# First three query tiles of an attention block: the value tiles become the stationary operand

## The reference

```
scores = q @ k.T / sqrt(64); keep = (key < n_sink) | (0 <= pos_q - pos_k < window)
a = exp(scores - max); a = a / (sum(a) + 1e-9); x = a @ v        # per head
h = max(x @ w_in, 0);  x = (h * h) @ w_out
h = x @ w2_in;  g = P(h) / Q(h);  out = g @ w2_out               # P, Q: polynomials in h and |h|
```

## Time and profile before

| | |
|---|---|
| median of 3 runs | 636.86 us (636.72 to 638.67) |
| profiled execution | 636.6 us, its span 634.9 us |
| PE busy | 625.2 us, 98% |
| DVE, ACT, POOL busy | 449.7, 380.2, 353.8 us (71%, 60%, 56%) |
| chain that ended last | PE 83%, DVE 12%, ACT 2%, POOL 1% |
| DMA over the span | 67 GB/s |

### The profile page before, as it was taken

One profiled execution on the slowest core, in us unless ns is written; L12 is line 12 of the kernel. 1 busy time (PEld: TensorE's weight loads), 2 busy tenths in 40 slices (PEclk: granted clock), 3 DMA queues, 4 the chain that ended last, 5 costly groups with the idle time before them and its releaser, 6 DMA issues.

```text
span 634.9 us, 10375 instructions
## 1 busy us (share of the span) xinstructions
PE 625.2 (98%) x3716; PEld 586.4 (92%) x3716; DVE 449.7 (71%) x705; ACT 380.2 (60%) x859; POOL 353.8 (56%) x431
## 2 busy tenths in 40 slices
PE   8999999999999999999999999999999999999997
PEld 6889999999999999999999998888999999999995
DVE  5655655354655656443567799998999989998995
ACT  4755666365444545443222576688777877778774
POOL 6899865122333334330222478777777677777773
PEclk9999999999999999999999999999999999999999
DMA  8776311052021401000444210021001110001001
GB/s 257 234 242 233 115 42 42 1 167 83 1 84 43 141 23 62 18 2 3 130 133 131 79 57 2 1 101 51 1 1 43 70 39 0 1 2 51 1 0 56
DMA packets 28972, 43.50 MB, mean 69 GB/s; under 512 B 4080, under 2 KB 19440, under 8 KB 28400
## 3 DMA queue, kind: packets, MB, share of 16 engines
q1 hardware_dynamic: 28912, 42.74, 20.7%
HBM read 36.44 MB, written 6.29 MB: 67 GB/s over the span
## 4 chain that ended last, share of the span: by engine, by line
PE 83%; DVE 12%; ACT 2%; POOL 1%; issue 1%; DMA 0%; DVEq 0%; ACTq 0%; POOLq 0%; SPq 0%
PE h_ps L1502 24%; PE y_ps L1514 20%; PE y_ps L1817 16%; PE s_ps L1502 8%; PE o_ps L1502 4%; DVE s_ps L1191 4%; PE o_ps L1629 3%; PE s_ps L1555 2%; DVE h_ps L1191 2%; PE s_ps L1577 2%; DVE p_buf L1194 2%; DVE p_buf L1185 1%; PE s_ps L1551 1%; DVE o_ps L1191 1%; PE y_ps L1551 1%
## 5 line engine op out<-in xcount | busy, mean ns | idle before, releaser
L1502 PE MATMUL h_ps<-xT,weights 128*128 128x384 f32 x960 | 190.1, 339 | 0.4 <-DVE sq L1201 0.3
L1502 PEld LDWEIGHTS h_ps<-xT,weights 128*128 128x128 f32 x960 | 167.3, 188 | 3.8 <-issue 2.5
L1514 PE MATMUL y_ps<-hid,weights 128*128 128x384 f32 x768 | 149.8, 338 | 0.0
L1817 PE MATMUL y_ps<-weights,hid 128*128 128x512 f32 x576 | 142.6, 393 | 1.3 <-POOL hid L765 0.8
L1514 PEld LDWEIGHTS y_ps<-hid,weights 128*128 128x128 f32 x768 | 132.9, 188 | 0.7 <-issue 0.7
L1817 PEld LDWEIGHTS y_ps<-weights,hid 128*128 128x128 f32 x576 | 106.8, 188 | 22.2 <-POOL hid L765 2.3
L845 ACT ACTIVATE sq<-sq 128x384 f32<-128x384 f32 x64 | 33.4, 522 | 103.1 <-DVE sq L1201 103.0
L765 POOL TENSOR_TENSOR hid<-p_buf,hid 128x384 fp32r<-128x384 f32 x63 | 65.7, 1043 | 42.9 <-ACT hid L1071 42.5
L1160 DVE TENSOR_TENSOR hid<-sq,hid 128x384 fp32r<-128x384 f32 x64 | 47.0, 734 | 59.7 <-ACT hid L803 59.7
L1191 DVE RECIPROCAL s_ps<-q_buf 128x384 f32<-128x384 f32 x32 | 82.0, 2561 | 3.3
L756 POOL TENSOR_TENSOR q_buf<-h_abs,q_buf 128x384 f32<-128x384 f32 x64 | 65.7, 1027 | 29.0 <-ACT q_buf L821 26.7
(11 more groups left out here) (147 smaller groups left out, 886.2 us busy)
## 6 DMA issues: line engine op xcount, KB each, us to landing
weights_raw<-in_w_pack SPq DMA_DIRECT2D x32, 512.0 KB, 4.3
bk_raw<-in_k_pack SPq DMA_DIRECT2D x24, 256.0 KB, 3.9
q_pair<-in_q_pack SPq DMA_DIRECT2D x21, 256.0 KB, 3.5
bv<-in_v_pack SPq DMA_DIRECT2D x24, 128.0 KB, 2.4
y_scratch<-xT SPq DMA_DIRECT2D x2, 1536.0 KB, 6.2
xT<-y_scratch SPq DMA_DIRECT2D x2, 1536.0 KB, 6.6
out_y<-out_stage SPq DMA_DIRECT2D x3, 768.0 KB, 3.6
inv_cols<-in_q_pack SPq DMA_DIRECT2D x3, 256.0 KB, 4.4
```

Source lines behind the costliest of these rows:

```text
L1502: ins = nc.tensor.matmul(bank, weights[:, i, wp, W_IN, t * P:(t + 1) * P], x, start=(t == 0 and n == 0), stop=(t == KC - 1 and n == 2))
L1514: ins = nc.tensor.matmul(y_ps[:, m, 0:NT], weights[:, i, wp, W_OUT, m * P:(m + 1) * P], hid[:, i % 2, gp, :], start=(i == 0 and n == 0), s ...
L1817: ins = nc.tensor.matmul(y_bank(turn, t), hid2[:, i % RING, gp, t * P:(t + 1) * P], weights[:, i, wp, W_OUT, :], start=(i == 0 and n == 0) ...
```

## The change

The first three tiles take the way of tiles 3 to 5. `weigh`, `finish`, both forms of `tile_out` and the semaphore `x_turned` go. PE weighs four heads in a burst in the turns 6, 10, 14, 18, 22 and 26, each one turn after the transposes of its last unit. After tile qt (`finished(s)` gives the tile and the turn within the next eight): DVE makes the inverse sums in turn 0, ACT spreads them in turn 1, PE transposes them in turn 2 behind the burst, ACT copies them in turn 3, DVE divides in turn 4, and ACT and DVE split in turn 5. The copied inverses and the divided tile lie in `sq`; the transposes go to the bank `y_ps[:, 2]`.

The loads of K for k = 4, 5 and of Q for k = 3 to 7 take 64 partition rows in place of 128 (the upper 64 rows of these queries are zeros and stay from earlier loads).

```diff
+        def finished(s):
+            return s // H - 1, s % H
+        def inv_place(qt):
+            return sq.rearrange("p r n -> p (r n)")[:, 0:DM] if qt < QT else inv_cols[:, :]
+        def inv_bank(qt):
+            return y_ps[:, 2, :] if qt < QT else s_ps[:, 0, :]
...
 load_k
-                sp.dma_start(bk_raw[:, heads_of(k), own_cols(k)], k_pack[k]).then_inc(k_loaded[k % 4], 16)
+                rows = slice(0, D if GROUP <= k < EARLY - 2 else P)
+                sp.dma_start(bk_raw[rows, heads_of(k), own_cols(k)], k_pack[k, rows]).then_inc(k_loaded[k % 4], 16)
 load_q
-                sp.dma_start(queries(k), q_pack[k]).then_inc(q_loaded[q_slot(k)], 16)
+                rows = slice(0, D if N_RING <= k < EARLY else P)
+                sp.dma_start(queries(k)[rows, :], q_pack[k, rows]).then_inc(q_loaded[q_slot(k)], 16)
...
 ACT, front
-                    for qt in split_at(s):
-                        tile_out(qt)
+                    qt, at = finished(s)
+                    if qt >= 0 and at == 1:
+                        spread(qt)
+                    if qt >= 0 and at == 3:
+                        inv_copy(qt)
+                    if qt >= 0 and at == 5:
+                        x_high(qt)
 DVE, front
-                    if s % H == 2 and s > H:
-                        finish(s // H - 1)
...
+                    if qt >= 0 and at == 0:
+                        sums(qt)
+                    if qt >= 0 and at == 4:
+                        divide(qt)
+                    if qt >= 0 and at == 5:
+                        x_low(qt)
 PE, front
-                    if 3 <= s < UNITS + 3:
-                        weigh(s - 3)
+                    if s % GROUP == 2 and GROUP < s < UNITS + GROUP:
+                        weigh_heads((s - GROUP) // H, [(s - GROUP) // GROUP % 2])
...
-                    for qt in done_at(s):
-                        tile_out(qt)
+                    qt, at = finished(s)
+                    if qt >= 0 and at == 2:
+                        turn_inv(qt)
```

More of the change, by code:

```diff
@@ L1243, in sums @@
                     dve.wait_ge(u_exp, H * (qt + 1))
-                    if qt > QT:
-                        dve.wait_ge(inv_spread, qt - QT)
+                    if qt:
+                        dve.wait_ge(inv_spread, qt)
                     nc.vector.tensor_scalar(row_den[:, :], row_sum[:, qt % 2, :], 1e-9, None, ALU.add
@@ L1249, in sums @@
                     nc.vector.reciprocal(row_inv[:, :], row_den[:, :]).then_inc(inv_made, 1)
[L1251 to L1262, removed]
                 def slot(s):
@@ L1584, in turn_p @@
                     ins.then_inc(u_turned, 1)
-                def weigh(u):
-                    qt, m, i = unit(u)
-                    k, g = u // GROUP, u // GROUP % 2
-                    wait_turned_copy(pe, u)
-                    if m % GROUP == 0:
-                        pe.wait_ge(bv_loaded[k % 4], 16 * (k // 4 + 1))
-                    if m == 0 and qt >= 2:
-                        pe.wait_ge(o_read, qt - 1)
-                    bank = o_bank(qt)
-                    last = turned_cols(u) // P - 1
-                    for t in range(1 if i == 0 else 2):
-                        at = turned_at(u) + t * P
-                        ins = nc.tensor.matmul(bank[:, D * m:D * (m + 1)], bpT[:, at:at + P],
-                                               bv[:, t, D * m:D * (m + 1)], start=(m == 0 and t == 0),
-                                               stop=(m == H - 1 and t == last), skip_group_check=True)
-                    if last == 2:
-                        if i == 2 and g == 0:
-                            pe.wait_ge(vs_loaded, 16 * (qt // KT + 1))
-                        heads = slice(GROUP * D * g, GROUP * D * (g + 1))
-                        ins = nc.tensor.matmul(bank[:, heads], bpT[:, 2 * GROUP * P:], bvs[:, heads],
-                                               start=False, stop=(g == 1), skip_group_check=True)
-                    ins.then_inc(u_pv, 1)
                 def weigh_heads(qt, groups):
-                    i = qt % KT
+                    i, bank = qt % KT, o_bank(qt)
                     first, last = H * qt + GROUP * groups[0], H * qt + GROUP * groups[-1] + GROUP - 1
@@ L1628, in weigh_heads @@
                             rows, at = slice(D * (h % 2), D * (h % 2) + D), (u % 2 * 2 + t) * P
-                            ins = nc.tensor.matmul(o_ps[rows, h // 2 * P:h // 2 * P + P], bv[:, t, D * h:D * (h + 1)],
+                            ins = nc.tensor.matmul(bank[rows, h // 2 * P:h // 2 * P + P], bv[:, t, D * h:D * (h + 1)],
                                                    turned_pair(u // 2)[:, at:at + P], start=(h < 2 and t == 0),
@@ L1638, in weigh_heads @@
                             rows = slice(D * (h % 2), D * (h % 2) + D)
-                            ins = nc.tensor.matmul(o_ps[rows, h // 2 * P:h // 2 * P + P], bvs[:, D * h:D * (h + 1)],
+                            ins = nc.tensor.matmul(bank[rows, h // 2 * P:h // 2 * P + P], bvs[:, D * h:D * (h + 1)],
                                                    turned_sinks(u), start=False, stop=(h >= H - 2),
@@ L1647, in slot, with turn_inv @@
                         turn_p(s - 2)
[L1648 to L1664 removed]
+                    if s % GROUP == 2 and GROUP < s < UNITS + GROUP:
+                        weigh_heads((s - GROUP) // H, [(s - GROUP) // GROUP % 2])
+                def turn_inv(qt):
+                    pe.wait_ge(inv_spread, qt + 1)
+                    if qt >= QT:
+                        wait_turned_copy(pe, H * qt + H - 2)
+                    elif qt:
+                        pe.wait_ge(inv_copied, qt)
+                    for c in range(KC):
+                        ins = nc.tensor.transpose(inv_bank(qt)[:, c * P:(c + 1) * P], o_sb[:, c * P:(c + 1) * P],
                                                   ident[:, :])
```

68 lines of the change are left out of this document (19 added, 49 removed).

## The result

The changed kernel takes 638.78 us (median of 13 runs, 638.54 to 640.64), the kernel before in the same rounds 636.22 (13 runs, 635.67 to 638.67): 1.0041 times as long, 95% interval 1.0033 to 1.0048. The forecast was +2.56 us, the difference of the medians is +2.56; as a time the forecast was 639.4, counted from a slower "before" of 636.86. So the change is slower, though by little more than the 0.3% that can be told from nothing.

The account below looks back on a forecast made before the run. PE was taken to bound the front, with little to spare on DVE and ACT. Terms -1.40 - 0.80 + 3.36 + 1.10 + 0.30 = +2.56 us gave 639.4 us, range for 8 in 10 from 635.0 to 641.4.

Parts of the forecast that it names:

- What bounds the front: Before the first feed-forward matmul: PE bounds; a shorter slot helps only while the round over DVE and ACT fits.
- PE's work and the waits for turned probabilities: Front: weighings save 2.60 us, six bursts cost 1.20, net -1.40; PE's waits before weighings go, -0.80.
- (a): Transposes of the inverse sums wait for ACT's spread: 0.98 us, then 0.42 for tile 1, none for tile 2; together 1.40.
- (b): Scores 16 and 24 wait for maxima queued on DVE behind `x_low`: 0.73 and 0.48 us, together 1.21.
- (c): The first feed-forward matmul waits for `x_low` of tile 2: 0.75 us.
- `x_low` itself: Now reading two SBUF sources while POOL works, up to 0.53 us longer each; two of three taken, +1.1 us.
- Smaller parts: Exponentials 14, 15, 22, 23 follow late maxima, so their transposes wait a little more, four times: +0.3 us (ends 0 and 0.8).
- The loads: Halved loads of K and Q, 0.9 MB less; PE does not wait for them: 0 us (ends -0.1 and 0).
- Rival 2: PE stays the bound, decided where (b) is zero at both tiles, with waits of (a) hidden: 634.4 us; chance 0.13.
- rival 3: Even result: waits half as long and `x_low` undisturbed, up to all waits without disturbance: 636.4 to 638.1 us; chance 0.28.
- Rival 4: Every `x_low` held 0.60 us, PE's 0.80 of waits stays, smaller waits at 0.8: +4.6, 641.2 us; chance 0.11.
- rival 1: Slower as summed: the round over ACT and DVE is longer than eight shorter slots; 639.4 us; chance 0.48.

Follow-up runs that it names:

- bursts_spaced: Kernel before with four-head weighing bursts and division one turn later, as bursts_only, plus tile output and split one turn later still (values not the reference's): 636.48 us.
- retimed: Changed kernel with tiles 0 and 1 turning the sums in turn 3, copying in 4, dividing in 5, splitting in 6 and 7: 637.25 us.
- low_late2: Same kernel as low_late, run once more (changed kernel with `x_low` of tiles 0 and 1 in turn 7 instead of 5): 638.18 us.
- in_psum: Changed kernel with the quotient of tiles 0 to 2 written back into its own PSUM bank, so `x_high` and `x_low` read PSUM: 638.22 us.
- tile2_early: Changed kernel with tile 2's round pulled forward one turn, its `x_low` staying in turn 5: 639.39 us.
- best_sbuf: retimed with tile 2's round also pulled forward one turn, as in tile2_early: 638.37 us.
- best: best_sbuf with the quotient written back into its PSUM bank: 637.59 us.
- full_loads: Changed kernel with whole 128-row loads of K and Q put back: 638.88 us.
- loads_only: Kernel before with only the 64-row loads of K (k = 4, 5) and Q (k = 3 to 7): 636.40 us.
- low_late: Changed kernel with `x_low` of tiles 0 and 1 in turn 7 instead of turn 5: 638.82 us.
- bursts_only: Kernel before with weighing in bursts of four heads and the old division one turn later (values of the first three tiles not the reference's): 637.55 us.

## Why the prediction was right, step by step

**What bounds the front: right.** PE had no free time, and a shorter slot was worth something only while the round over DVE and ACT fits in it. It doesn't: PE went from 0 to 3.23 us idle between 8 us and h. The signs named for "right" were there: h at 42.01, the waits at 14.64, 21.22 and 42.01, DVE idle for 1.19 to 1.22 us before each `x_low`.

**PE's work and the waits for turned probabilities, -2.20 forecast: off by 1.5.** PE's busy time up to h fell by 31.50 - 30.78 = 0.72; in bursts_spaced, with less waiting, by 1.18, in retimed by 1.55. The miss is not mainly in the weighings. Give each of PE's rows from 8 us to h the time up to the next start, without what is marked idle, and add them up by line (my sums from the two timelines, good to about 0.1 us):

| PE, 8 us to h | before | after |
|---|---|---|
| weighings and their sinks, with the fourth tile's first burst | 10.8 | 7.8 |
| scores | 13.5 | 13.8 |
| transposes of probabilities and of sinks | 5.8 | 7.6 |
| transposes of the divided tile or of the inverse sums | 1.3 | 1.5 |

The weighings came down by 3.0, where 2.60 and the 0.80 of waits before them were forecast: 0.4 short. The other rows took 2.3 more between them, 1.8 of it the transposes, where I had charged 1.20 for the bursts: 1.1 short. A burst costs 0.21 to 0.27 and not 0.20, at most 0.4 of that. Most of the rest fits the 15 transposes whose load waited for an exponential: the pair at 16.91 took 0.27 in place of 0.21, and such a delay stands in PE's busy time and not in its idle time. So the step that I had wrong was to let the other operations on PE keep their length while the round grew late.

**(a) `turn_inv`, 1.40 forecast:** 0.70, 0.16 and 0 on PE, 0.86 in all (PEld: 0.94, 0.41 and 0.17, close to the 0.98, 0.42 and 0 that I worked out). The links were right; PE itself had a little more cover, as its previous matmuls were still running. The 0.17 of tile 2 isn't a wait for the spread, but the gap behind a burst.

**(b) Scores 16 and 24, 1.21 and the lock:** 1.03 before score 16, 0.11 before score 24 (from 31.45 to 31.56). From score 11 to 16 it took 21.22 - 15.13 = 6.09 us; I had 5.50, with an undisturbed `x_low`, and that one took 1.14 and not 0.69, so 5.95. From score 19 to 24 31.56 - 25.39 = 6.17, forecast 6.05. The chains of links hold to about 0.15 us. The wait at score 24 came out 0.37 shorter than the 0.48 forecast because PE's own work in that stretch was put too short (5.57, where it took 6.06). The traces of low_late2 (4.89 for the stretch of 6.09) and in_psum (the wait halved) show in two ways that this place costs time.

**(c) `h_ps`, 0.75 forecast:** 0.66. From score 27 it took 42.01 - 36.17 = 5.84, forecast 5.68. tile2_early, best_sbuf and best took this wait away, and paid for it at `turn_inv`.

**`x_low` itself, 1.10 forecast: too much.** 1.14, 0.69 and 0.73: 0.49 over the undisturbed duration; in_psum, which takes it out, gained 0.56 by the median and 0.74 by h. One of three was hit, as in the earlier trace rows, and not two of three as I took it. POOL waited 3.3 us for weights, 2.2 of them in one piece, and the second `x_low` fell into that pause. How many are hit is chance of the order: with the same two sources it was two in full_loads (1.15 and 0.93) and none in retimed. The Trainium skill, "SBUF — State Buffer", "SBUF: two separate sides", has DVE and GpSimd locking each other out for a whole instruction, and names beside two SBUF inputs also DVE's two-port performance modes. The six rows of `row_den` above that took longer than 0.16 end within 0.03 us of POOL's operation, which agrees with the page, and they show that an operation of eight elements in each partition is held too.

**Smaller parts, 0.30 forecast: too little in kind.** Not four transposes but 15 had a load that waited for an exponential, 4.5 us of PEld against 0.8 before. What remains of PE's idle time is 3.23 - 0.86 - 1.03 - 0.11 - 0.66 = 0.57 us, of which 0.18 stand before such a transpose (28.60) and 0.16 before a score that waited for queries (8.39); the larger part of these waits is in the longer busy times above.

**The loads, 0:** right, by loads_only and full_loads.

So the idle time was forecast at 3.36 + 1.10 + 0.30 = 4.76 and came to 3.23, and the work at -2.20 and came to -0.72. The mechanism, its three places and the sign are shown; at score 24 hardly anything was waited. That the sum hit within 0.1 us is luck: two errors of 1.5 us, one in each direction.

Rival 2 (PE stays the bound) fell with the first trace. Its condition, a (b) of zero at both tiles, was nearly made true by retimed (0.22 before score 16), and even that is not below the kernel before: its 634.4 was too low because PE's busy time fell by 1.55 and not 2.20, and because 2.08 us of idle time stayed, 0.63 of it (c). The result lies above rival 3's range (636.4 to 638.1); retimed, the best order found, comes into it, still 1.0019 times before. Rival 4 kept PE's 0.80 of waits and dearer small parts, and these are where the forecast was too low, but the held `x_low` that it rested on was seen once in three. The rivals' times were counted from the profiled 636.6, while rival 1's had 0.26 added; this changes no reading.

## What to carry to other kernels

When an engine is full, ask what is behind it before you shorten its work: here the round of a unit over DVE and ACT only just fitted beside PE's work, so that bursts alone brought 0.1 us for 1.2 us of PE's busy time saved, and the operations added to the round came back as 2.7 us of waits in the places named. An operation that many later ones wait for should be laid a turn behind its source, and a latency chain should be moved as a whole: taking a turn out of the middle only moved the wait (0.63 before `h_ps` became 1.20 before `turn_inv`). A saving worked out for the shortened operation alone is not the engine's: here the weighings shrank by 3.0 us and PE's busy time by 0.7, since its other operations came to stand longer.

## What the runs showed of the hardware that I had not expected

- A DVE operation of almost no work (128 by 8, in SBUF) took between 0.16 and 1.00 us, and ended within 0.03 us of the POOL operation under way in each of the six rows above where it was held. Its place in the front is on the path to the spread sums.
- The lock holds both ways: POOL's subtractions of 128 by 256 took 0.73 us, and 1.17 for the one beside the `x_low` of 1.14.
- The granted clock was 0.79 from 8 to 16 us in two of the profiled executions (low_late and bursts_only), so below the upper level of 2.4 GHz for a part of the stretch, where PE had stood idle for 0.82 and 0.74 us shortly after 8 us, in low_late for the second load of keys. Microsecond by microsecond, low_late's clock was full up to 9, 0.59 from 9 to 10, 0.50 (the lower level of 1.2 GHz) from 10 to 12, 0.70 from 12 to 13, and full again from 13 on; PE had been busy for 0.18 of the us from 8 to 9. In low_late's repeat, with PE busy for 0.91 of that us, the clock was full. Score 11 started at 17.07 us against 14.90 in that repeat. An idle time of 0.51 us at the same place in best_sbuf left the clock full in its trace. Over all kernels here seven runs have a mean granted clock of 0.997, and each lies 0.7 to 2.4 us above its kernel's median; but there are long runs without it (641.48 in tile2_early, clock 0.999).
- Around a burst with a half-width stationary operand the loading of operands stood idle for 0.17 us on either side (17.88 to 19.27 in the changed kernel's trace; 0.17 to 0.20 at most of the other bursts).
